# The order of local and pooled attention work, and values three units late instead of two

## The reference

```python
q_d = q.reshape(B, H, Sd, 4, D).mean(axis=3)      # k_d, v_d likewise
out_d = sm_attn(q_d, k_d, v_d)                    # softmax attention over 144 pooled tokens
out_up = np.repeat(out_d, 4, axis=2)
mask = np.abs(pos[:, None] - pos[None, :]) < 4    # local: seven keys around each query
scores = np.where(mask, scale * (q @ k.T), -1e9)
out_local = softmax(scores) @ v
x = out_up + out_local                            # 2304 tokens x 512
...
h = x @ w_in; g = h * tanh(softplus(h)); x = g @ w_out
# then a second layer with softmax, layer norm and w_out
```

## Time and profile before

| what | value |
|---|---|
| runs | 691.76, 687.57, 689.03 us; median 689.03 |
| span of the profiled execution | 686.9 us |
| what lies between the median and that span | 2.1 us |
| PE, DVE, ACT, POOL busy over the span | 97, 62, 47, 41% |
| end of the attention stage on TensorE | 98.6 us |
| mean granted TensorE clock | 0.995 |

### The profile page before, as it was taken

The page is one execution under the profiler, slowest core; times in us unless marked ns, Lnnn a source line. Parts: engine busy times, 40 slices in busy tenths (PEclk is TensorE's granted clock), DMA queues, the critical chain, the costliest instruction groups (busy, mean ns, idle before and its releaser), DMA issues.

```text
span 686.9 us, 12938 instructions
## 1 busy us (share of the span) xinstructions
PE 667.5 (97%) x5002; PEld 573.1 (83%) x5002; DVE 425.9 (62%) x747; ACT 326.0 (47%) x687; POOL 284.2 (41%) x342
## 2 busy tenths in 40 slices
PE   6998899999999999999999999999999999999998
PEld 5777778888999989989899988888778888888886
DVE  7998759555765557555544412555788566766671
ACT  5998773233543446543443211137464454535441
POOL 6999713020694636645000000576435543354100
PEclk9999999999999999999999999999999999999999
DMA  8999692000000000000100001012100000000001
GB/s 259 247 262 262 157 336 114 0 1 1 0 1 1 1 1 1 1 1 1 62 1 2 1 0 35 27 31 63 31 17 16 31 32 31 8 25 31 32 16 46
DMA packets 26085, 37.52 MB, mean 55 GB/s; under 512 B 2484, under 2 KB 12714, under 8 KB 26026
## 3 DMA queue, kind: packets, MB, share of 16 engines
q1 hardware_dynamic: 26026, 36.71, 18.0%
HBM read 31.98 MB, written 4.72 MB: 53 GB/s over the span
## 4 chain that ended last, share of the span: by engine, by line
PE 89%; POOL 3%; DVE 2%; issue 2%; ACT 1%; DMA 1%; SPq 0%; POOLq 0%; DVEq 0%
PE psum L961 29%; PE psum L913 16%; PE psum L1074 13%; PE psum L1051 12%; PE psum L947 12%; PE psum L1060 2%; PE psum L813 1%; POOL prob L676 1%; PE psum L845 1%; PE psum L893 1%; DVE so L1768 1%; PE psum L832 1%; POOL half_qk L649 1%; DMA qkT<-kT_dram 1%; POOL half_v L659 1%
## 5 line engine op out<-in xcount | busy, mean ns | idle before, releaser
L961 PE MATMUL psum<-ghi,whi 128*128 128x512 f32 (+1 forms) x320 | 118.2, 370 | 0.0
L961 PE MATMUL psum<-glo,whi 128*128 128x512 f32 (+1 forms) x320 | 118.1, 369 | 0.0
L961 PE MATMUL psum<-ghi,wlo 128*128 128x512 f32 (+1 forms) x320 | 117.7, 368 | 0.0
L1210 ACT ACTIVATE g_sb<-psum 128x512 f32<-128x512 f32 (+1 forms) x48 | 25.3, 527 | 135.5 <-PE psum L913 134.7
L1586 DVE CAST ghi<-g_sb 128x512 fp32r<-128x512 f32 (+1 forms) x48 | 24.0, 500 | 101.8 <-PE psum L961 86.7
L913 PE MATMUL psum<-xhi,whi 128*128 128x512 f32 (+1 forms) x256 | 85.6, 365 | 0.5 <-ACT g_sb L1210 0.3
L1591 DVE TENSOR_TENSOR glo<-g_sb,ghi 128x512 fp32r<-128x512 f32 (+1 forms) x80 | 66.3, 829 | 19.6 <-ACT ghi L1236 17.9
L961 PEld LDWEIGHTS psum<-ghi,wlo 128*128 128x128 f32 x320 | 60.3, 189 | 10.2
L961 PEld LDWEIGHTS psum<-ghi,whi 128*128 128x128 f32 x320 | 60.5, 189 | 9.8 <-issue 0.4
L913 PE MATMUL psum<-xlo,whi 128*128 128x512 f32 (+1 forms) x192 | 68.0, 354 | 0.0
L961 PEld LDWEIGHTS psum<-glo,whi 128*128 128x128 f32 x320 | 60.5, 189 | 8.9
(11 more groups left out here) (175 smaller groups left out, 1618.7 us busy)
## 6 DMA issues: line engine op xcount, KB each, us to landing
wraw<-w_dram SPq DMA_DIRECT2D x12, 512.0 KB, 7.5
vw<-v_dram SPq DMA_DIRECT2D x30, 160.0 KB
qkT<-qT_dram SPq DMA_DIRECT2D x16, 288.0 KB, 4.0
qkT<-kT_dram SPq DMA_DIRECT2D x16, 288.0 KB, 5.7
out_dram<-ob SPq DMA_DIRECT2D x18, 256.0 KB, 2.0
v<-v_dram SPq DMA_DIRECT2D x16, 256.0 KB, 5.8
wraw<-w_dram SPq DMA_DIRECT2D x16, 256.0 KB, 6.8
b<-w_dram SPq DMA_DIRECT2D x4, 512.0 KB, 4.3
```

The lines of the kernel that those rows point to most:

```text
L961: ins = nc.tensor.matmul(psum[:, YB + m, 0:size], a[:, w], b[:, (t * F1 + f) % GR, 0:size], start=(f == 0 and n == 0), stop=(f == F1 - 1 a ...
L1210: nc.scalar.activation(g_sb[:, f % HR, 0:size], psum[:, HB1 + f % HB, 0:size], ACT.Mish).then_inc(g_ok, 1)
```

## The change

Work of one unit is ordered anew on every engine; no instruction of computation is added or left out. TensorE scores the local part first, turns the local part of u - 2, scores the pooled part, turns the pooled part of u - 2, and takes the values of u - 3 (BEHIND = 3). At step 14 it takes two units' values and is from then on two units late as before. ScalarE takes the local exponential ahead of the pooled one; VectorE subtracts the local maxima ahead of the pooled maxima, and keys or an eviction come ahead of both. GpSimd's and SyncE's work on v follows one step later. Two waits are new: turn_pooled for p_copied, value_pooled for od_ok. The tail is written out line by line. SOON is 12. (Blank context lines are left out.)

```diff
--- before.py
+++ after.py
@@ -407,14 +407,15 @@
             return 2 * (u // 2 + 1) + (1 if u % 2 == 0 or u == UNITS - 1 else 0)
         LATE = 2
-        FIRST = 2
+        BEHIND = 3
+        SOON = UNITS - BATCH
         AHEAD = 4
         W_IN = (13, 14, 15, 16)
-        ADDED = [c * BATCH + LATE + 1 for c in range(KD - 1)]
+        ADDED = [c * BATCH + BEHIND + 1 for c in range(KD - 1)]
         def flat(bank, width):
@@ -552,9 +553,9 @@
-            for s in range(UNITS + 3):
-                if 1 < s < UNITS + 2:
-                    u = s - 2
+            for s in range(UNITS + 4):
+                if 2 < s < UNITS + 3:
+                    u = s - 3
                     wait(sp, pool_v, u - 1)
                     sp.dma_start(v4[:, u % 2, :], v_d[u][0:POOLF * P].rearrange("(p t) c -> p (t c)", t=POOLF))\
                       .then_inc(ld_v4[u % 2], 16)
@@ -570,8 +571,8 @@
                     wait(sp, p_scored, s + 1 - RQ)
                     sp.dma_start(qkT[:, s % RQ, 0, 0:SEQ], qT_d[s]).then_inc(ld_qk[s % RQ], 16)
                     sp.dma_start(qkT[:, s % RQ, 1, 0:SEQ], kT_d[s]).then_inc(ld_qk[s % RQ], 16)
-                if s > 2:
-                    load_windows(s - 3)
+                if s > 3:
+                    load_windows(s - 4)
                 if s in W_IN:
                     load_w_in(0, W_IN.index(s))
             for kdx in range(KD):
@@ -681,10 +682,10 @@
                     normalise_local(u - 1)
                 if 0 < u + 1 < UNITS:
                     pool_queries_keys(u + 1)
-                if u < UNITS:
-                    pool_values(u)
-                    if u % 2 == 0:
-                        pool_two_tails(u)
+                if u > 0:
+                    pool_values(u - 1)
+                    if u % 2 == 1:
+                        pool_two_tails(u - 1)
                 if u == UNITS - 1:
                     pool.wait_ge(wi_hi, 2)
                     nc.gpsimd.tensor_tensor(first_low(1), in_piece(wraw, 1), first_high(1).bitcast(F32),
@@ -849,7 +850,8 @@
             def turn_pooled(u):
                 par = u % 2
                 pe.wait_ge(p_norm, u + 1)
-                wait(pe, od_ok, u)
+                wait(pe, p_copied, u)
+                wait(pe, od_ok, u - 1 if u < SOON else u)
                 for b in range(NPB):
                     at = b * PS
                     nc.tensor.transpose(turned[:, at:at + PR], pprob[0:PR, par, b, 0:P], ident[0:PR, 0:PR])
@@ -864,6 +866,7 @@
             def value_pooled(u):
                 par = u % 2
                 pe.wait_ge(p_copied, u + 1)
+                wait(pe, od_ok, u)
                 pe.wait_ge(pool_v, u + 1)
                 pe.wait_ge(pool_vt, u // 2 + 1)
                 half = slice(par * HD, (par + 1) * HD)
@@ -968,26 +971,37 @@
             pe.wait_ge(mask_ok, 4)
             pe.wait_ge(zero_ok, 1)
             pe.wait_ge(rest_ok, 5)
-            for u in range(UNITS + LATE):
+            for u in range(UNITS):
+                score_local(u)
                 if u >= LATE:
                     turn_local(u - LATE)
-                    turn_pooled(u - LATE)
-                if u < UNITS:
-                    if u >= FIRST:
-                        score_pooled(u)
-                    score_local(u)
-                    if u < FIRST:
-                        score_pooled(u)
-
-                if u == UNITS:
-                    pe.wait_ge(l_sub, UNITS)
-                if u >= UNITS:
-                    hidden(0, 2 * (u - UNITS))
-                if u >= LATE:
+                if u == SOON + LATE:
+                    value_pooled(SOON - 1)
+                    value_local(SOON - 1)
+                    turn_pooled(SOON)
+                    score_pooled(u)
+                else:
+                    score_pooled(u)
+                    if u >= LATE:
+                        turn_pooled(u - LATE)
+                if u >= SOON + LATE:
                     value_pooled(u - LATE)
                     value_local(u - LATE)
-                if u == UNITS:
-                    hidden(0, 1)
+                elif u >= BEHIND:
+                    value_pooled(u - BEHIND)
+                    value_local(u - BEHIND)
+            turn_local(UNITS - 2)
+            turn_pooled(UNITS - 2)
+            pe.wait_ge(l_sub, UNITS)
+            hidden(0, 0)
+            value_pooled(UNITS - 2)
+            value_local(UNITS - 2)
+            hidden(0, 1)
+            turn_local(UNITS - 1)
+            turn_pooled(UNITS - 1)
+            hidden(0, 2)
+            value_pooled(UNITS - 1)
+            value_local(UNITS - 1)
             for t in range(T1):
                 if t in FAST:
@@ -1242,37 +1256,50 @@
                     act.wait_ge(alo_ok, NPR * (FAST.index(t + 1) + 1))
                 nc.scalar.copy(xy[:, :, tile_tokens(t)], psum[:, YB:YB + KD, 0:SIZES[t]]).then_inc(y_ev, 1)
-            for u in range(UNITS + LATE):
-                if u >= LATE:
-                    copy_pooled(u - LATE)
-                    copy_local(u - LATE)
-                if 0 < u <= UNITS:
+            for u in range(SOON + LATE + 1):
+                if u >= BEHIND:
+                    copy_pooled(u - BEHIND)
+                    copy_local(u - BEHIND)
+                if u > BEHIND:
+                    evict_pooled(u - BEHIND - 1)
+                    if u % 2 == 0:
+                        evict_local(u - BEHIND - 1)
+                if u > 0:
                     normalise_pooled(u - 1)
-                if FIRST <= u < UNITS - 1:
-                    exp_pooled(u)
-                if u >= LATE:
-                    evict_pooled(u - LATE)
-                if u == UNITS - 1:
-                    exp_pooled(u)
-                    split_x(0, KD - 1)
-                    weights_in_high(1)
-                if u < UNITS:
-                    exp_local(u)
-                if u < FIRST:
-                    exp_pooled(u)
-                if LATE <= u < UNITS and u % 2 == 0:
-                    evict_local(u - LATE)
+                exp_local(u)
+                if u == SOON + LATE:
+                    evict_pooled(SOON - 1)
+                    copy_pooled(SOON)
+                    copy_local(SOON)
+                exp_pooled(u)
                 if u in ADDED:
                     split_x(0, ADDED.index(u))
-                if u == UNITS - 2:
-                    weights_in_high(0)
-                if u == UNITS:
-                    nc.scalar.preload_act_table_set("mish")
-                    mish(0, 0)
-                    for f in range(2, AHEAD):
-                        weights_in_high(f)
-                if u == UNITS + 1:
-                    mish(0, 1)
+            evict_pooled(SOON)
+            evict_local(SOON)
+            weights_in_high(0)
+
+            normalise_pooled(UNITS - 2)
+            exp_local(UNITS - 1)
+            copy_pooled(UNITS - 3)
+            copy_local(UNITS - 3)
+            exp_pooled(UNITS - 1)
+            evict_pooled(UNITS - 3)
+            split_x(0, KD - 1)
+            weights_in_high(1)
+
+            copy_pooled(UNITS - 2)
+            copy_local(UNITS - 2)
+            normalise_pooled(UNITS - 1)
+            evict_pooled(UNITS - 2)
+            nc.scalar.preload_act_table_set("mish")
+            mish(0, 0)
+            for f in range(2, AHEAD):
+                weights_in_high(f)
+
+            copy_pooled(UNITS - 1)
+            copy_local(UNITS - 1)
+            evict_pooled(UNITS - 1)
+            mish(0, 1)
             def weights_two_in(n):
                 act.wait_ge(ld_w2in, 64)
@@ -1547,20 +1574,15 @@
                 nc.vector.tensor_tensor(first_low(f), in_piece(wraw, f), first_high(f).bitcast(F32),
                                         ALU.subtract).then_inc(wi_lo, 1)
-            for u in range(UNITS + LATE):
-                if u < UNITS:
-                    if u >= FIRST:
-                        maxima_pooled(u)
-                    subtract_local(u)
-                    if u < FIRST:
-                        maxima_pooled(u)
-
-
-                if LATE <= u != UNITS - 1 and (u % 2 == 1 or u >= UNITS):
-                    evict_local(u - LATE)
-                if u < UNITS - 1:
-                    if u % 2 == 0:
-                        pool_keys(u + 1)
+            for u in range(UNITS):
+                if BEHIND < u < SOON + LATE and u % 2 == 1:
+                    evict_local(u - BEHIND - 1)
+                if u % 2 == 0 and u < UNITS - 1:
+                    pool_keys(u + 1)
+                subtract_local(u)
+                if u == SOON + LATE:
+                    evict_local(SOON - 1)
+                maxima_pooled(u)
                 if u in ADDED:
                     add_pooled(0, ADDED.index(u))
                 if u - 1 in ADDED:
@@ -1568,16 +1590,15 @@
                 if u == UNITS - 1:
                     weights_in_low(0)
                     split_x(0, KD - 1)
-                if u < UNITS:
-                    sum_local(u)
```

(13 more changed lines are left out.)

## The result

| | before | after |
|---|---|---|
| median of six runs each, us | 687.85 (685.30 to 691.76) | 698.75 (695.59 to 700.45) |
| ratio, 95% interval | | 1.0147 (1.0126 to 1.0168) |
| profiled execution: time, span, us | 689.03, 686.9 | 697.94, 696.1 |
| first product of the feed-forward part, us | 85.96 | 94.75 |

The account below looks back on a forecast made before the run. No engine was taken as alone at its limit: all four 92 to 96% busy, GpSimd most. A feed-forward start 0.5 us late plus 1.5 for the clock gave +2.0 on 689.0, so 691.0 us, range 686 to 696.

Parts of the forecast that it names:

- S(14): End of VectorE's subtraction of unit 14: forecast 74.5 us, between 73.7 and 75.1, a gain of 2.2.
- Start: First units: pooling unit 1's keys first makes unit 0's subtraction end at 9.22, 1.3 us later, regained by unit 2.
- The ring: VectorE and ScalarE waiting on each other in the steady units: 4.70 us per unit, 4.04 without keys or eviction.
- 1.7 us of cover: TensorE's steady units: local scores start 0.7 late behind the pooled turn's wait, with 1.7 us to spare; cost 0.
- Additions and splits: VectorE's adds and splits of x, 0.6 us each, between maxima and sum, where it would stand 0.43: cost 0 to 0.2.
- GpSimd: GpSimd's work in the attention stage: 4.83 us per unit on average, normalisations 3.6 and 5.8 apart in turn.
- The end: TensorE catches up a unit from unit 14: stall 2.7 us, feed-forward start 86.5, 0.5 late, plus 1.5 for the clock.
- Rival 4: Steady units longer than the start shows, by 0.3 us per unit over 11 units: +3.3, 694.3 us; chance 13%.
- Rival 3: TensorE's short stands in each unit lower the clock in the middle: 8 us for three units, 697 to 699; chance 7%.
- Rival 1: The end closes up or the middle runs at 4.70; stall under 1 us, clock stays: about 686.8 us; chance 17%.
- the middle case: The forecast case for the whole kernel: +2 us within 1.5, around 691.0; chance 45%.

Follow-up runs that it names:

- the kernel with both cuts: Changed kernel with a third buffer for local probabilities and TensorE's pooled scores ahead of both turns: 694.9 us, ratio 1.0077.
- The third buffer: Changed kernel with three instead of two buffers for local probabilities, so VectorE's subtraction waits for an earlier local turn: 698.65 us, ratio 1.0134.
- the scores ahead of the turns: Changed kernel with TensorE scoring the pooled part ahead of the local turn: 698.48 us, ratio 1.0136.
- moving the cast: Changed kernel with ScalarE's rounding of x moved from ahead of the copies to behind the next unit's copies: 698.06 us, ratio 1.0121.
- The copies ahead of the exponential: Changed kernel with ScalarE doing the copies and od eviction of unit 13 ahead of unit 15's local exponential: 694.55 us, ratio 1.0077.
- VectorE and ScalarE alone: Kernel before with only VectorE and ScalarE taking local work ahead of pooled, od evicted behind both exponentials, TensorE's order kept: 712.51 us, ratio 1.0341.
- all four edits together: Changed kernel with third probability buffer, pooled scores ahead of turns, x's rounding behind the copies, unit 13's copies first at the end: 691.53 us, ratio 1.0035.
- the kernel with thin loads: Kernel with all four edits, loading one of five blocks of v windows from unit 2 on: 688.83 us; kernel before, loaded likewise: 684.58 us.

## Why the prediction was wrong

The forecast for S(14) was 74.5 and for the start of the feed-forward part 86.5 + 1.5 = 88.0; they were 79.99 and 94.75. Of the 6.75 us between, 5.5 were lost in the middle and 1.25 at the end.

**Start: right.** S(0) was forecast at 9.22 and came at 9.31, S(2) near 18 and came at 18.05.

**The ring: the step that failed.** That "the ring is 2.05 + 0.37 + 0.66 + 0.80 + 0.82 = 4.70 us" holds (S(1) to S(2) took 4.70, and the kernel with both cuts repeats it), but it was not the longest ring. In the paragraph on TensorE I looked for what is queued behind the pooled turn's new wait, and found "1.7 us of cover". I didn't ask the same of the local turn. It needs the local copy of the part before, for which ScalarE has its place behind the pooled exponential; the pooled scores are queued behind it, and the subtraction needs it through the two prob buffers. S(3) was 0.94 late, 0.85 of it by that (4.89 instead of 4.04 from S(2)), and the five plain units behind it took 4.97, 4.89, 4.98, 4.89 and 4.97, 1.2 more than five times 4.70. The third buffer (no change in the time), the scores ahead of the turns (4.88) and both (4.70) show it.

**Additions and splits: mis-sized.** "I cost them at 0 to 0.2", since VectorE would stand for 0.43 there. VectorE did stand, nine times for 0.36 to 0.61 at dsum, and as forecast not where x is added. But the six units concerned took 32.35 together, 4.15 more than six times 4.70. 2.50 of that are in the three units with an addition: the split has a half on ScalarE, ahead of the copies, and that is in the ring; moving the cast brought the first two to the length of the others. 1.65 are in the three with a rest of x, where the subtraction waits for nobody: VectorE's split took 1.15, 0.99 and 0.78 instead of the 0.6 priced, which is more than the stand of 0.43 hides, and in the last keys landed 0.27 late. I followed only VectorE's half of the moved step, and priced that at its shortest.

**GpSimd: right that it would not bind** beyond its average; it waited for rden seven times, up to 3.6 us. The 3.6 and 5.8 between normalisations became 4.0 to 4.9 and 5.7 to 6.1 in turn, as the units themselves were longer.

**The end: right in kind, short by 1.25.** Counted from S(14), the pooled maxima, exponentials and evictions came at 2.8, 3.6 and 4.7 as forecast. The addition in front of unit 15 took 1.63 instead of 0.6 (GpSimd normalised and halved v at the same time), so S(15) came at 8.87, not 7.9, and the copy of 13 at 10.2, not 9.3. The stall was 3.09 against 2.7. Behind it 4.5 us went by for values and both turns, which I had at 2.7: 1.8 for the clock against 1.5 charged, and 0.4 more behind 94.75. The copies ahead of the exponential (4.2 us back) show the stall and the clock; the addition's length was not tested by itself.

**Two sums** are off by a little: 19.5 / 4 is 4.88, and only 19.3 gives 4.83, and 7.9 + 0.65 + 0.64 is 9.2, not 9.3. Neither moves the forecast by more than 0.3.

**The rivals.** Rival 4, a ring longer than its start shows, was right in kind; its price of 0.3 a unit was right for plain units, and it left out the additions: 3.3 stood for what became 5.5 with S(3)'s part. Rival 3 didn't come: the clock was 1.00 from 20 to 80 us, though TensorE stood in every unit, so what the Trainium skill says of short pauses between groups of matmuls ("TensorE: Matmul & The Clock Gate", A second HAM failure mode) doesn't show here; once the stage is under way before and after show a low clock only at stalls of 2.41 and 3.09 us. Where TensorE stood 1.98 us in every unit (VectorE and ScalarE alone) the granted clock was 0.92 from 20 to 80, so a lower clock in the middle did come there, with waits longer than the ones forecast here. Rival 1's two conditions can be had by hand, a closed end and a ring at 4.70: all four edits together gave 691.5, not the 686.8 that it promised. Pauses on TensorE are 2.7 of the difference, by the kernel with thin loads (688.8); the rest is VectorE's additions and the end, S(14) to S(15).

**The range** added the ring's uncertainty at 0.3 a unit to the middle case only. Rival 4 on top of the forecast's low clock and end gives 694.3 and had 13%; a second miss of the same sign, the 4.15 of the additions, was in none of the cases.

**What stays open.** That the pauses are waits for TensorE's instructions is shown by the packets. That data in the DMA engines is what delays those packets is argued, not shown: they start earlier and the pauses go when the loads are thinned, but anything which thins the loads also moves the units against each other. A kernel that keeps the full loads and only places them around those counts was not tried. Open is also what a mended end would give: the only kernel that tried it brought no gain.

## What to carry to other kernels

When an order is changed, list for each buffer that exists once or twice who frees it, and follow that chain around all the in-order engines until it comes back; the longest such ring sets the unit, and a wait that seems covered can hold the work queued behind it. A moved helper that records on two engines must be costed on both. If an experiment cuts one ring and nothing changes, read which wait is now there before giving the theory up: two rings of nearly equal length hide each other.

## What the runs showed of the hardware

TensorE paused in the middle of groups behind the same counts of instructions in kernels of different order, some 248 recorded ones apart, for 0.2 to 2.94 us, and went on 1.3 to 1.8 us behind the end of a 16 KB packet on the DMA queue for instructions. The share of the DMA engines from 20 to 80 us says only roughly how bad it gets: at 0.87 to 1.02 single pauses reached 1.8 to 2.94 us; at 0.74 and 0.85 one of 1.0 came all the same; in the kernel after (0.82) there were none of 0.15 or more, and with few windows (0.67, 0.64) those of the late units went. The Trainium skill, "Runtime: NRT & Kernel Launch", Instruction fetch mechanics, says that instructions are fetched in blocks of 256 and that crossing a block is mostly hidden; the packet's size and the spacing agree with the block, and by these runs the crossing is not hidden when the packet starts late. The kernel before became 5.2 us faster with thinner loads. So a faster middle packs the same bytes into less time and can pay some of the gain back in such pauses.

One stall does not always cost the clock. The same wait of 2.16 us at the first turn of a local part was followed by a granted clock of 0.69 from 21 to 26 us in the kernel with the cast moved, and by 1.00 in those with the third buffer and with the end reordered; 3.09 and 3.10 us at the end came with a low clock each time, and 2.38 us, a pause in the kernel with both rings cut, with none (1.00 from 72 to 88). The six runs of the kernel after differ by it: mean clock 1.000 with a span of 693.7, 0.995 with 696.1, 0.990 with 698.6. So the clock behind a stall of some 2 us is a price of 0 to 2 us, not a number.

VectorE's addition of two SBUF tiles took 0.69, 1.27 and 1.63 us in the same kernel. GpSimd halved v beside the one of 1.27 (both from 69.79), and normalised and halved v beside the one of 1.63; beside one of 0.69 (49.30) it was GpSimd's halving that took long, 1.28 instead of 0.72. The earlier trace rows show the same for its half sum. That one of the two holds up the other is read from these overlaps and was not tested.
